# Attention of a chunk in one visit of TensorE: the next chunk's scores behind the outputs, half of y in free columns of the MLP's banks

## The reference

```python
# 1. linear attention: batch 4, 8 heads, 768 positions, 48 columns a head
for t in range(S):
    cur = einsum('bhd,bhe->bhde', u * k[t], v[t])
    y[t] = einsum('bhd,bhde->bhe', r[t], state + cur)
    state = w * state + einsum('bhd,bhe->bhde', k[t], v[t])
# 2. MLP on 3072 tokens: 384 -> 2048 -> 384
h = x @ w_in
z = maximum(0.01 * h, h) @ w_out
# 3. mixture of 8 experts, top 1, with a skip gate
do = z @ w_skip > 0; e = argmax(z @ w_gate)
out = z + gate * (relu(z @ w1[e]) @ w2[e])   where do, else z
```

## Time and profile before

| what | us |
|---|---|
| median of three timed runs (lowest, highest) | 669.46 (668.72, 670.49) |
| the profiled execution's own time | 666.72 |
| its span | 665.0 |
| TensorE busy with matmuls (share) | 646.2 (97%) |
| VectorE busy | 401.4 (60%) |
| ScalarE busy | 309.5 (47%) |
| GpSimd busy | 86.0 (13%) |

### The profile page before, as it was taken

The page is one execution under the profiler, slowest core; times in us unless marked ns, Lnnn a source line. Parts: engine busy times, 40 slices in busy tenths (PEclk is TensorE's granted clock), DMA queues, the critical chain, the costliest instruction groups (busy, mean ns, idle before and its releaser), DMA issues.

```text
span 665.0 us, 14201 instructions
## 1 busy us (share of the span) xinstructions
PE 646.2 (97%) x4733; PEld 606.9 (91%) x4734; DVE 401.4 (60%) x867; ACT 309.5 (47%) x683; POOL 86.0 (13%) x102
## 2 busy tenths in 40 slices
PE   8989999999999999999999999999999989999994
PEld 7878999999999999999999999999999879989993
DVE  7876765656656575466555545653466854865752
ACT  5466534345334443454434344333346435746650
POOL 5240000100010001001000100010021141423311
PEclk9999999999999999999999999999999999999998
DMA  8935625220422321242114221201505267686300
GB/s 226 301 130 205 212 72 174 73 71 18 134 68 71 96 75 54 64 143 73 48 30 139 73 72 30 76 8 57 213 1 206 92 199 277 207 284 264 130 21 8
DMA packets 39325, 78.09 MB, mean 117 GB/s; under 512 B 9032, under 2 KB 27494, under 8 KB 39216
## 3 DMA queue, kind: packets, MB, share of 16 engines
q1 hardware_dynamic: 34272, 62.96, 30.2%
q10 hardware_dynamic: 2432, 9.76, 4.3%
q0 software_dynamic: 2560, 4.58, 2.2%
HBM read 61.68 MB, written 13.00 MB: 112 GB/s over the span
## 4 chain that ended last, share of the span: by engine, by line
PE 89%; DVE 3%; ACT 2%; issue 2%; DMA 1%; POOL 1%; SPq 0%; ACTq 0%; POOLq 0%; DVEq 0%
PE bank L808 31%; PE bank L831 30%; PE bank L908 8%; PE bank L925 7%; PE bank L673 3%; PE bank L735 3%; PE bank L742 2%; PE bank L756 1%; PE bank L916 1%; DMA stage<-in_rk_t 1%; PE bank L865 1%; PE bank L901 1%; ACT am L1100 1%; PE bank L716 0%; DMA zg<-z_rows,get 0%
## 5 line engine op out<-in xcount | busy, mean ns | idle before, releaser
L1138 ACT ACTIVATE h_sb<-bank 128x384 f32<-128x384 f32 x128 | 62.8, 491 | 221.6 <-PE bank L808 221.4
L1448 DVE TENSOR_TENSOR h_sb<-h_sb,bank 128x384 f32<-128x384 f32 x128 | 70.9, 554 | 156.2 <-ACT h_sb L1138 156.2
L808 PE MATMUL bank<-x_hi,win_hi 128*128 128x384 f32 x384 | 135.1, 352 | 1.0 <-DVE win_lo L1494 0.6
L831 PE MATMUL bank<-wout_hi,g_hi 128*128 128x394 f32 x384 | 132.0, 344 | 0.4 <-DVE state L1424 0.4
L831 PE MATMUL bank<-wout_hi,g_lo 128*128 128x394 f32 x384 | 131.2, 342 | 0.0
L831 PE MATMUL bank<-wout_lo,g_hi 128*128 128x394 f32 x384 | 131.1, 342 | 0.0
L808 PE MATMUL bank<-x_hi,win_lo 128*128 128x384 f32 x384 | 129.5, 337 | 0.0
L808 PE MATMUL bank<-x_lo,win_hi 128*128 128x384 f32 x384 | 129.3, 337 | 0.0
L1455 DVE TENSOR_TENSOR g_lo<-h_sb,g_hi 128x384 fp32r<-128x384 f32 x128 | 71.8, 561 | 30.7 <-ACT g_hi L1145 29.7
L1145 ACT ACTIVATE g_hi<-h_sb 128x384 fp32r<-128x384 f32 x128 | 66.7, 521 | 42.3 <-DVE h_sb L1448 40.9
L1927 POOL DMA_INDIRECT id_list<-idgate,dst x24 | 24.4, 1016 | 449.0 <-DVE dst L1655 444.1
(11 more groups left out here) (250 smaller groups left out, 895.5 us busy)
## 6 DMA issues: line engine op xcount, KB each, us to landing
raw<-in_experts SPq DMA_DIRECT2D x32, 768.0 KB, 6.0
rkt<-in_rk_t SPq DMA_DIRECT2D x46, 192.0 KB, 3.7
rkn<-in_rk_nat SPq DMA_DIRECT2D x21, 384.0 KB, 4.4
v<-in_v_nat SPq DMA_DIRECT2D x24, 192.0 KB, 3.0
z_rows<-z_sb SPq DMA_DIRECT2D x24, 192.0 KB, 2.8
out<-z_sb SPq DMA_DIRECT2D x24, 192.0 KB, 2.8
stage<-in_win ACTq DMA_DIRECT2D x4, 768.0 KB, 4.5
stage<-in_wout_t ACTq DMA_DIRECT2D x4, 768.0 KB, 6.6
```

The lines of the kernel that those rows point to most:

```text
L808: mm = pe.matmul(h_ps[t % 2][:, 0:GT], a[:, kk, cols], b[G % 2][:, kk, :], start=n == 0, stop=n == 3 * KT - 1)
L831: mm = pe.matmul(z_ps[i][:, 0:ZW], a[t % 3][:, tok], b[:, f, :], start=f == 0 and j == 0, stop=f == FT - 1 and j == 2)
L1138: act.activation(h_sb[t % 2][:], h_ps[t % 2][:, 0:GT], ACT.Copy, scale=SLOPE).then_inc(s_h_scaled, 1)
L1448: dve.tensor_tensor(h_sb[t % 2][:], h_sb[t % 2][:], h_ps[t % 2][:, 0:GT], ALU.max).then_inc(s_leaky, 1)
```

## The change

Attention gets one visit a chunk. `ENDS[n]` is now the step of `state_sums(n)` and `outputs(n)`: 2, 6, 10 for chunks 3 to 5 as before, then 15, 20, 25, next 31, 36, 41 and so on, one step later than before. For chunks above 5 (JOINED) the scores are run at the step of the outputs of the chunk in front, right behind them. `rank` moves to the head of its step, in front of them. The state sums of chunks from 5 on, and the ranks, go to free columns of `y_ps`; the half q = 1 of y goes to columns 384 to 511 of the two hidden banks. ScalarE's copy of y is split: `out_y_front` (y_ps and one of the hidden banks) and `out_y_rest` (the other), the second behind high_g. Masks, scaling, diagonals and splits get new steps.

```diff
+JOINED = 2 * CPG - 1
+ENDS = {CPG + i: 4 * i + 2 for i in range(CPG)}
+ENDS |= {CPG * (G + 1) + i: FT * G - 1 + 5 * i for G in range(1, GROUPS - 1) for i in range(CPG)}
+BEGIN = {n: ENDS[n] - 2 if n <= JOINED else ENDS[n - 1] for n in ENDS}
-SPLIT_AT = {BEGIN[n] + (4 if n == 5 else 5): n for n in BEGIN}
+SPLIT_AT = {ENDS[n] + (2 if n == JOINED else 3): n for n in ENDS}
+DIAG_AT = {BEGIN[n] - 2 if n <= JOINED else BEGIN[n]: n for n in ENDS if n > CPG}
+MASK_AT = {BEGIN[n] if n <= JOINED else BEGIN[n] + 2: n for n in ENDS}
...
 def sums_in(n):
+            return a_ps[0] if n < JOINED else y_ps[:, 2 * P:]
+        def y_part(n, q, c):
+            if n < JOINED or q == 0:
+                return y_in(q)[:, P * c:P * c + P]
+            return h_ps[(ENDS[n] + c) % 2][:, GT:GT + P]
 def ranks_in(G):
-            return late_ranks if G == LATE else a_ps[1]
+            return late_ranks if G == LATE else y_ps[:, 2 * P + PAIRS * D:]
...
 # TensorE
+            def y_bank_free(n):
+                if n <= JOINED:
+                    pe.wait_ge(s_y_out, n)
+                else:
+                    pe.wait_ge(s_y_front, n - JOINED)
+                pe.wait_ge(s_state_done, min(max(n, CPG), CHUNKS - B))
+                if CPG < n <= 2 * CPG:
+                    pe.wait_ge(s_wg_lo, n - CPG + 1)
+                if n in RANKED_BEFORE:
+                    pe.wait_ge(s_slot, RANKED_BEFORE[n] + 1)
 def outputs(n):
+                for q in range(2):
+                    if q == 1 and n >= JOINED:
+                        pe.wait_ge(s_y_out, n)
+                        pe.wait_ge(s_leaky, ENDS[n] + 2)
+                    for p in range(PAIRS):
...
 def gate_products(q):
-                    pe.wait_ge(s_y_out, CPG + q)
+                    if CPG + q <= JOINED:
+                        pe.wait_ge(s_y_out, CPG + q)
+                    else:
+                        pe.wait_ge(s_y_front, 1)
+                        pe.wait_ge(s_state_done, CPG + q)
 def hidden(t):
+                n = ENDS_AT.get(t - 3)
+                if n is not None and n >= JOINED:
+                    pe.wait_ge(s_y_front, n - JOINED + 1)
+                n = ENDS_AT.get(t - 4)
+                if n is not None and n >= JOINED:
+                    pe.wait_ge(s_y_out, n + 1)
...
 for step in range(STEPS):
+                if step > FT and step % FT == 4:
+                    rank(step // FT - 1)
+                n = ENDS_AT.get(step)
+                if n is not None:
+                    if n >= JOINED:
+                        y_bank_free(n)
+                    if n < CHUNKS - B:
+                        state_sums(n)
+                    outputs(n)
                 n = BEGUN_AT.get(step)
                 if n is not None:
                     scores(n)
-                n = BEGUN_AT.get(step - 2)
-                if n is not None:
-                    if n < CHUNKS - B:
-                        state_sums(n)
-                    outputs(n)
-                if step > FT and step % FT == 4:
-                    rank(step // FT - 1)
...
 # ScalarE
+            def out_y_front(n):
+                act.wait_ge(s_y_done, n + 1)
+                act.wait_ge(s_x_in, 160 * (n - CPG))
+                act.activation(y_sb[:, 0:2, :]..., y_ps[:, 0:2 * P], ACT.Copy)
+                act.activation(y_sb[:, 3, :], y_part(n, 1, 1), ACT.Copy).then_inc(s_y_front, 1)
+            def out_y_rest(n):
+                act.wait_ge(s_leaky, ENDS[n] + 3)
+                act.activation(y_sb[:, 2, :], y_part(n, 1, 0), ACT.Copy).then_inc(s_y_out, 1)
 # its step, n = ENDS_AT.get(step):
+                    out_y_front(n)          # n >= JOINED, in front of scale_h
                     scale_h(step + 2)
+                n = DIAG_AT.get(step - 1)
+                    set_diag(n, range(4, H))
                     high_x(n)               # SPLIT_AT
                     high_g(step + 2)
+                    out_y_rest(n)           # n >= JOINED
+                n = DIAG_AT.get(step)
+                if n is not None and n > JOINED:
+                    set_diag(n, range(4))
...
 # VectorE, its step: leaky, routing, MASK_AT, low_x (SPLIT_AT), then for n > JOINED
+                n = BEGUN_AT.get(step + 4)  # scale_r(n), scale_k(n)
+                n = BEGUN_AT.get(step + 2)  # multiply_ruk(n)
+                n = BEGUN_AT.get(step + 1)  # scale_kn(n), sum_diag(n)
+                n = ENDS_AT.get(step)       # update_state(n)
 # update_state(n >= JOINED) and take_ranks(G < LATE) also wait for s_y_front
 # SyncE: move_y(n), load_v(n + 2) at ENDS[n]
```

More of the change, by code:

```diff
@@ L428, in sums_in @@
         def sums_in(n):
-            return (y_ps, y_ps[:, PAIRS * D:], z_ps[1])[n] if n < CPG else a_ps[0]
+            if n < CPG:
+                return (y_ps, y_ps[:, PAIRS * D:], z_ps[1])[n]
+            return a_ps[0] if n < JOINED else y_ps[:, 2 * P:]
         def rows_in_bank(n):
@@ L723, in outputs @@
                 v_loaded(pe, n)
[L724 to L737, removed]
+                if n < JOINED:
+                    y_bank_free(n)
[4 more added lines that the diff above has]
+                    for p in range(PAIRS):
+                        h = 2 * p + q
+                        first = p < 2 or q == 1 and n >= JOINED
+                        mm = pe.matmul(y_part(n, q, p // 2)[64 * (p % 2):64 * (p % 2) + 64],
+                                       v_of(n)[:, D * h:D * h + 64], am[q][:, p, :],
+                                       start=first, stop=n // B == 0, skip_group_check=True)
                 if n // B > 0:
@@ L741, in outputs @@
                             rows = slice(64 * q, 64 * q + 64)
-                            mm = pe.matmul(y_in(q)[64 * (p % 2):64 * (p % 2) + 64, P * (p // 2):P * (p // 2) + P],
+                            mm = pe.matmul(y_part(n, q, p // 2)[64 * (p % 2):64 * (p % 2) + 64],
                                            state[batch(n)][rows, p, :], rt[n % 2][rows, p, :],
@@ L1249, in _ @@
                     load_stage(LOADED["wout", step // 4 + 1])
+                n = ENDS_AT.get(step)
+                if n is not None and n >= JOINED:
+                    out_y_front(n)
                 if step + 2 < STEPS:
@@ L1254, in _ @@
                     set_diag(3, range(H))
-                n = BEGUN_AT.get(step - 2)
-                if n is not None:
-                    out_y(n)
-                n = BEGUN_AT.get(step + 2)
-                if n is not None and n > CPG:
-                    set_diag(n, range(4))
-                n = BEGUN_AT.get(step + 1)
-                if n is not None and n > CPG:
+                if n is not None and n < JOINED:
+                    out_y(n)
+                if DIAG_AT.get(step) in (4, 5):
+                    set_diag(DIAG_AT[step], range(4))
+                n = DIAG_AT.get(step - 1)
+                if n is not None:
                     set_diag(n, range(4, H))
@@ L1272, in _ @@
                     high_g(step + 2)
+                n = ENDS_AT.get(step)
+                if n is not None and n >= JOINED:
+                    out_y_rest(n)
+                n = DIAG_AT.get(step)
+                if n is not None and n > JOINED:
+                    set_diag(n, range(4))
                 if step in (3, 7, 11):
@@ L1720, in _ @@
             for step in range(STEPS):
-                if SPLIT_AT.get(step - 1) == 5:
-                    low_x(5)
+                if SPLIT_AT.get(step - 1) == JOINED:
+                    low_x(JOINED)
                 if step in (1, 5, 9):
@@ L1729, in _ @@
                     route_spots(step // FT - 1)
-                n = BEGUN_AT.get(step)
+                n = MASK_AT.get(step)
                 if n is not None:
@@ L1733, in _ @@
                 n = SPLIT_AT.get(step - 1)
-                if n is not None and n != 5:
+                if n is not None and n != JOINED:
                     low_x(n)
-                n = BEGUN_AT.get(step + 4)
-                if n is not None and n >= POOLED:
-                    multiply_ruk(n)
                 n = BEGUN_AT.get(step + 3)
-                if n is not None and n > CPG:
+                if n is not None and CPG < n <= JOINED:
                     sum_diag(n)
@@ L1743, in _ @@
                 n = BEGUN_AT.get(step + 2)
-                if n is not None and n > CPG:
+                if n is not None and CPG < n <= JOINED:
                     scale_k(n)
+                n = BEGUN_AT.get(step + 4)
+                if n is not None and n > JOINED:
+                    scale_r(n)
+                    scale_k(n)
+                n = BEGUN_AT.get(step + 2)
+                if n is not None and n > JOINED:
+                    multiply_ruk(n)
                 n = BEGUN_AT.get(step + 1)
@@ L1748, in _ @@
                     scale_kn(n)
-                n = BEGUN_AT.get(step - 2)
+                if n is not None and n > JOINED:
+                    sum_diag(n)
+                n = ENDS_AT.get(step)
                 if n is not None and n < CHUNKS - B:
```

23 lines of the change are left out of this document (13 added, 10 removed).

## The result

| | before | after |
|---|---|---|
| median of 20 runs each (lowest, highest), us | 668.65 (667.07, 671.37) | 670.98 (668.97, 673.67) |
| profiled execution, its span, us | 666.72, 665.0 | 671.03, 669.2 |
| TensorE busy, us | 646.2 | 645.2 |
| from the start of project(9) to that of project(127), us | 444.25 | 446.69 |

The ratio after to before is 1.0036, with a 95% interval of 1.0023 to 1.005: the change costs about 2.4 us (1.5 to 3.3). A second comparison of the same two kernels, on another occasion, gave 1.0043 (1.0030 to 1.0056), or 2.0 to 3.7 us. The forecast was +1.5 us and 671.0; that 671.0 and 670.98 agree so closely is luck, since the kernel before came out 0.8 us faster over 20 runs than over the first three, and the change cost 0.9 us more than forecast by the last row of the table.

A forecast was written before the change was run, and what follows sets the result against it. TensorE, busy 646.2 of 665.0 us, was taken as the bound. Terms -4.0 + 3.2 + 1.6 + 0.7 = +1.5 us, added with rounding to the timed median of 669.46, gave 671.0 us, range 666.6 to 673.8.

The forecast's parts named there:

- Joined scores: TensorE: scores of 18 chunks behind the preceding chunk's outputs save 0.19 us each, a drain staying inside; -3.4 us.
- Rival B: TensorE's joined visit: no drain between state products and scores, 3.1 us more saved, 667.9 us; chance 0.14.
- Ranks: TensorE: six ranks moved from visits of their own into the outputs' visit save 0.11 us each; -0.6 us.
- Z behind the diagonals: ScalarE at six group ends: set_diag before out_z makes TensorE's next project late by 0.53 us each; +3.2 us.
- Low_x behind leaky: VectorE, six groups' last chunks: low_x behind leaky delays the next group's first hidden by 0.26 us each; +1.6 us.
- Gate products: Step 10/11, once: gate_products(3) waits for update_state(5), behind leaky and low_x(4) on VectorE; +0.7 us.
- Moved at no cost: Moved loads, y's later copy and ten DMAs, masks and scaling stay hidden; high_x has 0.8 us to spare.
- Rival A: Copies of z and low_x come in time, only step 11 stalls: -3.3 us, 666.2 us; chance 0.14.
- rival C: Rank waits for VectorE's routing, 3 us if VectorE is 0.5 us late: +4.5, 674.0 us; chance 0.15.

The follow-up runs named there:

- e5_own_visit: e3_both with the joining alone undone: scores of chunks 6 to 23 in a visit of their own, one step later; ratio 0.9994 to the kernel before.
- e7_quarters: e3_both with the joined scores in 16 matmuls of 64x64 tiles instead of 8 of 64x128; ratio 0.9912 to the kernel before.
- e1_diag_ahead: Changed kernel with the first four set_diag back between scale_h and high_g in ScalarE's steps 15, 31, ..., 95; ratio 0.9987 to the kernel before.
- e4_all_diag_late: Changed kernel with all eight set_diag, not four, in front of out_z in ScalarE's steps 15, 31, ..., 95; ratio 1.0172 to the kernel before.
- e2_low_x_ahead: Changed kernel with low_x of a group's last chunk in front of leaky in VectorE's step, not behind it; ratio 1.0020 to the kernel before.
- e6_early: e3_both with update_state(5) at the head of VectorE's step 10 and low_in(3) behind leaky in step 9; ratio 0.9943 to the kernel before.
- e8_all: e3_both with the edits of e6_early and e7_quarters together; ratio 0.9902 to the kernel before.
- e9_chain: e8_all with high_g and out_y_rest in front of ScalarE's high_out(3), low_x(5) in front of VectorE's low_g(14); ratio 0.9905 to the kernel before, median 660.33 us.
- e3_both: Changed kernel with the edits of both e1_diag_ahead and e2_low_x_ahead; ratio 0.9946 to the kernel before.
- e10_after_again: The changed kernel run and profiled once more, unedited; ratio 1.0043 to the kernel before, project(9) to project(127) 446.63 us.

## Why the prediction was right

- **Joined scores, -3.4.** Right, in size and cause. L764 to L685 took the forecast 0.60 us, e5_own_visit measured 0.18 a chunk against 0.19 (for 17 of the 18), and e7_quarters showed that the 0.17 us between them go with the change of tile shape. Rival B (no drain) is refuted. The Trainium skill's rule (TensorEngine Tiling (Array Packing), Key Properties), that a change of tiling mode drains TensorE and a change of tile does not, held: in the visits the pauses are 0.12 to 0.26 us where the shape changes and absent where it does not. Their size is no constant of the two shapes: in front of L778 it is 0.25 or 0.26 behind the 394 columns of L863 and 0.03 behind the 24 columns of rank.
- **Ranks, -0.6.** Mis-sized. Not tested alone, but e5_own_visit has everything of the change but the joining, and against the kernel before, its intervals with a rank and the outputs beside it are together 0.26 us shorter over the six. From project(12) to project(127) it is 1.07 us shorter in all; the other 0.8 are hundredths in the steps around each visit, which the forecast did not have.
- **Z behind the diagonals, +3.2.** Right in mechanism, by e1_diag_ahead and the dose of e4_all_diag_late; measured 3.6. The first copy ended 0.04 us before the forecast time, but TensorE started 0.145 us behind its end, where the sum had 0.04.
- **Low_x behind leaky, +1.6.** Right in mechanism, by e2_low_x_ahead; measured 2.2. Low_x ended where forecast, but from its end to L840's start are 0.147 us, and I had put 0.05 for the semaphore. This hand-over, a tenth of a microsecond too small twelve times, is about the whole of the 1.0 us by which the two terms were short.
- **Gate products, +0.7.** They waited 0.75, of which 0.55 remained. Missed was leaky(11), for which the outputs in step 10 wait: VectorE ran it behind low_in(3), and the outputs stopped for 0.5 us. I took the q = 1 wait as met from a step without weight splits.
- **Moved at no cost.** This held in the changed kernel, but chunk 5's chain from y to x_lo was not costed for the first group, where its slack was the smallest: it cost 0.8 to 1.6 us in e4_all_diag_late, e6_early, e7_quarters and e8_all, for the most part by DMAs that landed 0.5 to 1.9 us more slowly than the 1.8 of the forecast. The prediction had named slower landings as what would eat this slack.
- **Rival A** (the covers hold) is refuted by the twelve lags, **rival C** (rank late) did not occur in the changed kernel; in e9_chain one rank started 0.7 us late.

The sum was -4.0 + 5.5 = +1.5; measured are -4.4 + 6.85 = +2.44 in the trace. The sum stayed near because its two errors have opposite signs: the savings were 0.4 us larger, the losses 1.35 larger. The change did save what its joined visits could save and lost more to two queue positions. With these two mended (e3_both) it is 0.5% faster than the kernel before, with square quarters as well 0.9%.

## What to carry to other kernels

When the bound engine's stream is made shorter, write out the in-order queues of the others for the step in which a handover falls: 1.27 us of work on an engine that is idle half the time cost TensorE 0.6 us a time in front of the copy that it waits for (the slack ate the rest), the next 1.27 us cost 1.17, and two places earlier they cost nothing. Measure stalls of a few tenths from start to start, not from a table of waits. Group TensorE's small matmuls by tile shape, and where a product can take its neighbour's shape, try that shape: here it gave 0.2 us a visit.

## What the runs showed of the hardware

**A microsecond or two at the start come and go with the single execution.** In the profile of the changed kernel TensorE's granted clock (the third figure from the right) fell after an idle stretch, here with its stretches of 2 us, the first with no TensorE work at all:

```profile
36.00:38.00 2.00, 0.00 (x0) 0.00 (x0) 0.98 (x2) 2.00 (x6) 0.94 (x1) 1.00 1.01 209
38.00:40.00 2.00, 1.49 (x32) 1.52 (x32) 2.00 (x3) 1.08 (x2) 0.00 (x0) 0.89 1.03 402
40.00:42.00 2.00, 1.77 (x8) 1.40 (x6) 2.00 (x5) 0.53 (x1) 0.43 (x1) 0.50 0.15 58
42.00:44.00 2.00, 2.00 (x10) 2.00 (x10) 1.32 (x2) 0.44 (x2) 1.92 (x2) 0.75 0.00 0
```

At 0.50, the lower of the two levels, 1.2 GHz, eight matmul records lie where the kernel's second profile, e10_after_again, has 11:

```profile
36.00:38.00 2.00, 1.37 (x8) 1.06 (x7) 1.49 (x3) 2.00 (x4) 0.44 (x1) 1.00 1.02 290
...
40.00:42.00 2.00, 1.86 (x11) 1.90 (x12) 2.00 (x4) 0.55 (x2) 0.94 (x1) 1.00 0.05 18
```

The first project to the third took 12.4 us there, 9.4 in e10_after_again, 10.4 before and 10.3 to 10.8 in all other profiles. The clock is a part of this alone. Up to the attention visit between them TensorE waited 2.52 us for VectorE's `am` in the first, 0.64 in e10_after_again and 1.53 in e3_both; without these waits the three are 9.8, 8.7 and 8.9, so the fall cost 1.0 us and the longer wait 1 to 2. In e6_early the clock fell from 34 to 38 us, and the distance was 10.4 as elsewhere: the slow matmuls filled the time in which the other kernels waited for `am`. E1_diag_ahead and e4_all_diag_late had a fall from 14 to 22 us (0.50 from 15 to 20), and in both project(0) started at 35.3 and 35.1 us instead of 30.7 to 33.5. All of this lies in steps that the edits do not touch. What sets it off is not shown.

The mean granted clock of each execution is on record, and the times go with it: of the changed kernel's 20 executions the five at 0.991 took 672.8 to 673.7 us, the nine at 0.996 or 0.997 took 669.0 to 671.1. By the medians of the two groups that is 2.3 us, half of the spread of 4.7 us between this kernel's executions. And 1.8 us of the 4.3 that separate the two first profiles are not the change's.

**Four tiles of 64x64 load side by side.** 32 such loads took 0.92 us, 0.03 apart, 16 loads of 64x128 took 0.97, 0.06 apart.

**From the end of the last write to TensorE's start** were 0.145 us behind ScalarE's z copies and 0.146 to 0.148 behind VectorE's low_x where a matmul waited for them, in the changed kernel.
